# A delta-rule attention with two feed-forward nets on one core: stage 0 with six banks and an order of its own, part of the weight work on GpSimd, and group 1's columns in stage 1

## The reference

```python
k_n = k / (np.linalg.norm(k, axis=-1, keepdims=True) + 1e-06)
for t in range(S):                       # B, H, S, D = 4, 8, 768, 48
    kt, vt, bt = (k_n[:, :, t], v[:, :, t], beta[:, :, t, None])
    y[:, :, t] = np.einsum('bhd,bhde->bhe', q[:, :, t], state)
    v_old = np.einsum('bhde,bhd->bhe', state, kt)
    state = state + bt[:, :, :, None] * np.einsum('bhd,bhe->bhde', kt, vt - v_old)
...
h = np.maximum(x @ w_in, 0.0)            # x: 3072 tokens x 384, w_in: 384 x 2048
x = h * h @ w_out                        # w_out: 2048 x 384
...
gate = 1.0 / (1.0 + np.exp(-(x @ w_gate)))
val = x @ w_val                          # 384 x 1536 each
return gate * val @ w_out                # 1536 x 384
```

## Time and profile before

| | |
|---|---|
| device time, three runs | 1011.26 us median (1009.72 to 1011.65) |
| profiled execution | 1009.18 us |
| its span, from the first to the last instruction | 1007.4 us |
| PE busy | 959.8 us, 95% of the span |
| DVE, ACT, POOL busy | 543.9, 481.2, 13.3 us |
| mean granted TensorE clock, as a share of full speed | 0.974 |

### The profile page before, as it was taken

One profiled execution on the slowest core, in us unless ns is written; L12 is line 12 of the kernel. 1 busy time (PEld: TensorE's weight loads), 2 busy tenths in 40 slices (PEclk: granted clock), 3 DMA queues, 4 the chain that ended last, 5 costly groups with the idle time before them and its releaser, 6 DMA issues.

```text
span 1007.4 us, 23469 instructions
## 1 busy us (share of the span) xinstructions
PE 959.8 (95%) x10030; PEld 490.9 (49%) x10030; DVE 543.9 (54%) x1075; ACT 481.2 (48%) x865; POOL 13.3 (1%) x27
## 2 busy tenths in 40 slices
PE   2876999999999999999999999999999999999997
PEld 1463565565565456546544444444444444444443
DVE  7979957947857885793335532523423423424322
ACT  4875575756576477555669732232222222221321
POOL 0000000000000000000000000000000000000000
PEclk7868999999999999999999999999999999999999
DMA  9516016015005202202033010010100100100000
GB/s 312 120 35 127 2 34 128 33 49 113 33 4 109 50 34 65 64 33 77 21 126 126 1 63 1 0 62 0 62 0 0 62 0 0 62 0 0 31 0 31
DMA packets 20708, 52.16 MB, mean 52 GB/s; under 512 B 2640, under 2 KB 12880, under 8 KB 20240
## 3 DMA queue, kind: packets, MB, share of 16 engines
q1 hardware_dynamic: 20032, 50.60, 17.8%
q10 hardware_dynamic: 592, 0.33, 0.2%
HBM read 41.48 MB, written 9.44 MB: 51 GB/s over the span
## 4 chain that ended last, share of the span: by engine, by line
PE 87%; DVE 6%; ACT 2%; issue 2%; DMA 1%; SPq 0%; POOL 0%; DVEq 0%; POOLq 0%
PE psum L641 75%; PE psum L555 2%; PE psum L499 1%; PE psum L486 1%; DMA raw_a<-in_w_in 1%; PE psum L512 1%; PE psum L524 1%; DVE attn L1086 1%; PE psum L542 1%; ACT w L822 1%; PE psum L570 1%; PE psum L584 1%; DVE work L1127 1%; PE psum L451 1%; DVE attn L1066 1%
## 5 line engine op out<-in xcount | busy, mean ns | idle before, releaser
L641 PE MATMUL psum<-work,attn 128*128 128x512 f16 x1944 | 419.9, 379 | 0.1
L641 PE MATMUL psum<-work,w 128*128 128x512 f16 x1728 | 386.3, 380 | 9.7 <-issue 5.9
L641 PEld LDWEIGHTS psum<-work,attn 128*128 128x128 f16 x1944 | 190.1, 98 | 229.7 <-DVE work L1127 0.6
L641 PEld LDWEIGHTS psum<-work,w 128*128 128x128 f16 x1728 | 164.2, 98 | 204.5 <-issue 9.5
L728 ACT ACTIVATE work<-work 128x512 f16<-128x512 f32 (+1 forms) x264 | 155.7, 624 | 142.9 <-DVE work L1260 139.9
L1260 DVE SCALAR_TENSOR_TENSOR work<-psum,work 128x512 f32<-128x512 f32 x72 | 49.8, 692 | 271.4 <-PE psum L641 261.8
L728 ACT ACTIVATE work<-psum,scal 128x512 f32<-128x512 f32 x90 | 60.5, 686 | 169.9 <-PE psum L641 169.9
L1108 DVE SCALAR_TENSOR_TENSOR work<-work 128x512 f16<-128x512 f16 x96 | 66.1, 690 | 61.5 <-ACT work L728 59.8
L728 ACT ACTIVATE attn<-psum 64x384 f32<-64x384 f32 (+5 forms) x160 | 65.9, 441 | 65.8 <-PE psum L512 34.7
L728 ACT ACTIVATE work<-psum 128x512 f32<-128x512 f32 x96 | 57.2, 595 | 64.3 <-PE psum L641 63.0
L1066 DVE TENSOR_TENSOR attn<-attn 128x31 f32<-128x31 f32 (+15 forms) x186 | 63.8, 343 | 6.4
(11 more groups left out here) (97 smaller groups left out, 558.5 us busy)
## 6 DMA issues: line engine op xcount, KB each, us to landing
attn<-in_kt SPq DMA_DIRECT2D x24, 192.0 KB, 4.2
attn<-in_v SPq DMA_DIRECT2D x24, 192.0 KB, 4.6
attn<-in_kn SPq DMA_DIRECT2D x24, 192.0 KB, 3.8
x_spill<-work SPq DMA_DIRECT2D x6, 768.0 KB, 3.4
xt<-x_spill SPq DMA_DIRECT2D x6, 768.0 KB, 5.0
y_out<-work SPq DMA_DIRECT2D x6, 768.0 KB, 3.6
attn<-in_qt SPq DMA_DIRECT2D x20, 192.0 KB, 4.1
work<-in_w_out SPq DMA_DIRECT2D x1, 3072.0 KB, 23.7
```

Of the source, the lines that this page charges most:

```text
L641: m = mm(dst, x, z, start=first and i == 0, stop=last and i == len(a) - 1)
```

## The change

Stage 0 gets a table of its own. The pool has six banks there instead of three: the three further ones are PSUM banks 2, 3 and 4, which the pieces of `w_in` and later the outputs use too (`a_bank`, `PIECE_SHARED`). A bank goes to a fill by longest rest, and the read-out of three fills is put later than the fill (`READ_LATER`). The 12 pieces of `w_in` go four by four into the same four banks, with group 1's Grams of keys between them. `cut_out` and `cut_small`, eight instructions, go from ACT to GpSimd. `place_e` is done by halves. The maximum of x is taken chunk by chunk, and ACT makes the high part of group 0's x. `start` of stage 0 is 35, so that `coefficients`, `start_lanes` and all 31 columns of group 1 come behind `split_x`. `keep_clock` stands behind certain fills (`WARM_BEHIND`) instead of ahead of them.

```diff
+NB_FIRST = 6
...
-    0: dict(mid=(2, 2), off=(8, 15), qk=(7, 19), ks=(-7, 14), dr=(13, 20), grow=(14, 25), xt=(14, 28), xmax=28, xscale=31, xsplit=31, kk=(0, 0), lanes=5, norm=6, start=8, small=(3, 7, 17, 17), hi_out=(0, 4, 8, 9), first_out=(7, 8, 19, 21)),
+    0: dict(kk=(0, 1), qk=(2, 9), mid=(3, 5), off=(4, 7), dr=(6, 13), grow=(8, 14), ks=(-7, 10), xt=(11, 15), lanes=3,
+            norm=3, root=12, xmax=16, xscale=17, xsplit=18, start=35, place_e=(3, 8), first_out=(5, 7, 13, 13), first_max=13),
...
+READ_LATER = {("qk", 0, 1, 0): 12, ("qk", 0, 1, 1): 12, ("off", 0, 0, 1): 9}
...
+    _n = NB_FIRST if _s == 0 and (_kind, _g) != ("kk", 1) else NB
+    _b = min(range(_n), key=lambda b: _last[b])
...
-REST_BANK, REST_PIECES = (2, 3, 4, 1, 5, 6, 7, 2, 3, 4, 1, 2), 12
-REST_FIRST = 12
+REST_PIECES = 12
+REST_BANK = (1, 3, 4, 2) * 3
+REST_AT = {OPEN: (0, 1, 2, 3), 0: (4, 5, 6, 7), 1: (8, 9, 10, 11)}
...
+WARM_BEHIND = {("mid", 0, 0): 4, ("mid", 1, 1): 1, ("dr", 1, 1): 4, ("su", 1, 1): 2, ("xt", 1, 1): 14}
...
-        a_bank = [psum[:, b, :] for b in (5, 6, 7)]
+        a_bank = [psum[:, b, :] for b in (5, 6, 7, 2, 3, 4)]
...
             def open_fill(*f):
 
+                if f in PIECE_SHARED:
+                    pe.wait_ge(w_lo_done, REST_PIECES)
...
+            def first_high_parts():
+
+                act.wait_ge(x_scaled, 5)
+                act.wait_ge(w_small_done, W_PIECES)
+                act.wait_ge(w_out_done, W_PIECES)
+                for kc in range(KC):
+                    run(x_hi[:, kc], xt32[:, TOK * kc:TOK * (kc + 1)], scale=cell(X + 2)).then_inc(x_cut, 1)
...
+            def cut_out(n):
+
+                at = slice(part // W_PIECES * n, part // W_PIECES * (n + 1))
+                nc.gpsimd.tensor_scalar(w1h[:, 2 * part:3 * part][:, at], raw_o[:, at], cell(WO + 2), None, ALU.mult)\
+                    .then_inc(w_out_hi, 1)
...
             all_of(wsq_part, wsq_all, 2, WO, RADD)
+            pool.wait_ge(w_step, W_STEPS * 2)
+            for n in range(W_PIECES):
+                cut_out(n)
+            pool.wait_ge(small_scaled, 1)
+            for n in range(W_PIECES):
+                cut_small(n)
...
+            def max_of_chunk(c):
+
+                for x in range(2):
+                    wait_taken(dve, "xt", 0, c, x)
+                link(V.tensor_reduce(scal[:, 32 + KC * c:32 + KC * (c + 1)],
+                                     xt32[:].rearrange("p (k c f) -> p k c f", k=KC, c=NC)[:, :, c], AX.X, ALU.max,
+                                     apply_absolute_value=True), xmax_first, c + 1)
```

More of the change, by code:

```diff
@@ L116, in other_work @@
 def other_work(s, step):
-    us = sum(EVACUATION.get(kind, 0.0) for kind, *_ in FILL_AT.get((s, step), []))
+    us = sum(EVACUATION.get(kind, 0.0) for kind, *_ in READ_AT.get((s, step), []))
     for name, cost in (("rows", 4.3), ("scale_v", 3.2), ("xmax", 1.8), ("xscale", 1.0), ("xsplit", 4.0), ("lanes", 2.2),
@@ L622, in attention @@
                         turn(g, c, x)
+                    if s == 0:
+                        keep_clock(WARM_BEHIND.get((kind, c if kind not in ("mid", "off") else x, x), 0) if g == 0 else 0)
             def rest_of_first(n):
@@ L678, in stage @@
                     attention(s, step)
[L679 to L683, removed]
+                    if s == 0:
+                        for n in REST_AT.get(step, ()):
                             rest_of_first(n)
@@ L891, in stage @@
                     if 0 < s < GROUPS and step == place(s, "rows") + 1:
-                        place_e(s)
-                    for f in FILL_AT.get((s, step), []):
+                        place_e(s, slice(0, UN), NC)
+                    for f in READ_AT.get((s, step), []):
                         evacuate(*f)
+                    if s == 0 and step in place(0, "place_e"):
+                        c = place(0, "place_e").index(step)
+                        place_e(0, slice(PAIRS * c, PAIRS * (c + 1)), 1)
+                    if s == 0 and step == place(0, "xsplit"):
+                        first_high_parts()
                     if s == 0 and step == OPEN:
@@ L905, in stage @@
                         weight_root(1, WO)
-                        for n in range(REST_FIRST):
+                    if s == 0:
+                        for n in REST_AT.get(step, ()):
                             cut_rest_first(n)
-                    if s == 0 and step == 0:
-                        place_e(0)
-                    for n in range(REST_FIRST, REST_PIECES):
-                        if s == 0 and step == place(0, "rest")[n - REST_FIRST]:
-                            cut_rest_first(n)
-                    for n in range(W_PIECES):
-                        if s == 0 and step == place(0, "hi_out")[n]:
-                            cut_out(n)
-                        if s == 0 and step == place(0, "small")[n]:
-                            cut_small(n)
-                    if s < GROUPS - 1 and step == place(s, "norm"):
+                    if s < GROUPS - 1 and step == place(s, "norm" if s else "root"):
                         root_k(s + 1)
@@ L1203, in stage @@
                         scale_v(s)
-                    for f in FILL_AT.get((s, step), []):
+                    for f in READ_AT.get((s, step), []):
                         evacuate(*f)
+                    if s == 0 and step == place(0, "first_max"):
+                        max_of_chunk(0)
                     if chain and step == place(s, "xmax"):
```

68 lines of the change are left out of this document (39 added, 29 removed).

## The result

The changed kernel takes 1030.1 us (median of 4 runs, 1029.2 to 1031.2) where the kernel before took 1010.7 beside it: a ratio of 1.0183, 95% interval 1.0171 to 1.0195. It is slower, as I had said, but by 19.5 us and not by 4, and it lies outside my range. The profiled execution has a span of 1026.4 us and a time of 1030.21, so 3.8 us lie outside its span, where it was 1.8 before; the three other executions have spans of 1027.2 to 1029.1 us. Medians that are compared with this kernel's therefore differ by some 2 us more than the fixed points in the traces do.

The account below looks back on a forecast made before the run. PE (TensorE) was taken as the bound, busy nearly throughout, so only an earlier F pays: -4.5 + 8.25 = +3.8 us on the profiled 1009.2 gives 1013.0, with 2.1 to the median 1015; range 1008.5 to 1024.

Parts of the forecast that it names:

- F: Start of TensorE's first hidden block, 93.18 us in the kernel before; forecast at 88.7 us, a gain of 4.5.
- Term 2: Stage 1, behind F: 11.2 us of VectorE's coefficients and columns move there, making TensorE wait 8.25 us.
- The wait for the keys and its cold clock: Stage 0: TensorE idles 5.9 us from 32.3 for group 1's keys, then half clock costs 3.3 us, between 0 and 4.
- Rival A: At 38 us in stage 0 the clock costs nothing: F = 85.4, 1011.7 us, no change; chance 0.19.
- The parts that cost nothing: Stage 0: GpSimd's eight pieces at 1.6 us each, between 1.43 and 3.6, decide only above 5.6; ACT's relief and six banks add nothing.
- Rival B: Stage 0: GpSimd's reads each stop one VectorE column; F = 91.7, 1018 us, or 1024 at 2.2 us each; chance 0.28.
- term 1: Stage 0 walk along PE's and DVE's new order: F = 85.4, or 88.7 with 3.3 us for the clock.
- Rival C: Stage 0: PE not held at group 1's keys; F = 82.7, 1009.1 us; chance 0.16 with a too-long walk added.

Follow-up runs that it names:

- experiment 1: The changed kernel with the eight pieces of w_out back on ScalarE (ACT) instead of GpSimd; 1020.25 us, ratio 1.0092.
- experiment 3: experiment 1 with group 1's coefficients and first nine columns back in stage 0; 1012.32 us, ratio 1.0009.
- experiment 8: The changed kernel with each of GpSimd's eight pieces written as two instructions of 768 elements; 1029.08 us, ratio 1.0173.
- experiment 7: experiment 3 with the edits of experiment 5 and experiment 6 together; 1006.54 us, ratio 0.9948.
- experiment 6: experiment 3 with 19 more zero products ahead of chunk 1's first products, where TensorE stands still at 70 us; 1010.17 us, ratio 0.9989.
- experiment 5: experiment 3 with group 1's keys loaded ahead of values, queries and the k*s keys in SP's queue; 1008.76 us, ratio 0.9973.
- experiment 4: The kernel before with the eight pieces of w_out on GpSimd and the small scale made earlier; 1035.72 us, ratio 1.0242.
- experiment 10: experiment 7 with halved pieces on GpSimd, an idle all-reduce behind them, group 1's lanes cleared between the two sets; 1008.48 us, ratio 0.9979.

## Why the prediction was wrong, point by point

The sign was right and the size was not: 8.25 us of debt were there, and the gain of 4.5 ahead of F was a loss of 10.7.

- **Term 2, the debt of 8.25 us: right.** 8.3 in the changed kernel, 7.9 from experiment 1 to 3. The first `project` starts at F + 11.1, forecast as F + 11.2, and the block behind group 1's first `mid` at F + 39.4, forecast as about 40. How the time is spent differs: the wait ahead of that `project` is 3.4 us and not 5 to 6, because the three hidden blocks ahead of it ran cold and ended at F + 7.7 and not at F + 5.9. The added waits are 6.2 us (5.3 for the low parts, 0.9 for the attention), and the first five blocks take 1.9 us longer than before (13.07 us for 11.16).
- **The wait for the keys and its cold clock: right.** The keys' products began at 39.16 and not 38.2, and the first `qk` started at 55.72 where the walk, with the clock's 3.3 us, has 51.5 + 3.3 = 54.8: 0.9 late, all of it from the keys. Rival A (no cost of the clock) is out.
- **"The parts that cost nothing" is the step that failed.** It priced the pieces at 1.6 us within 1.43 to 3.6 and said that they decide only above 5.6. They took 4.3 to 4.5, outside both bounds and still under 5.6, and the price was not what mattered. What did was a cost that I had not on the list: changing GpSimd to another kind of instruction and back, 6.4 to 7 us each in this kernel, the second time between the maximum of x and the split. It put 6.65 us on F; the holds put 1.2 there. Without the pieces the change takes 1020.25 us (experiment 1), still 5 us over the forecast; that rest is the walk and the second cold stretch, below.
- **Rival B** had the mechanism right (VectorE held by GpSimd's reads) and the victims only in part. It had each piece stop one column; in fact one column, the scaling of v, one small instruction of one input, and the first two of the four low pieces of `w_out` were held, for longer each, and the path saw 1.2 us and not 6.3 to 12.5. The Trainium skill's page "SBUF — State Buffer", section "Who interferes with whom", says that the engine that comes second is blocked until the other's instruction is done, for VectorE instructions with two SBUF inputs and also for `tensor_scalar` in a two-port mode. The traces agree, with 3.26 us for 60 elements and 2.16 for a TENSOR_SCALAR of 32 that takes 0.19 alone (whether this one ran in such a mode no view shows); experiment 8 agrees on the length.
- **The walk itself, term 1, was too short by 4.2 us.** With no cold stretch on the way and no pieces on GpSimd (experiment 7) it is 90.91 - 52.84 = 38.1 us from the first `qk` to F, where my walk has 85.4 - 51.5 = 33.9. Of this, 2.0 are two `qk` fills, which I took at 1.1 us like the other kinds and which take 2.08 at full clock; the other 2.2 are spread over the steps behind. That every fill costs 1.1 was a choice, and no row of `qk` was read for it, though the trace of the kernel before has one at full clock:

```profile
75.36 2.08 PE L486 MATMUL psum<-attn 48*64 48x64 f32 x64
```

- **The second cold stretch was missing: 2.2 us** (experiment 6). My walk had a wait ahead of `qk` of chunk 1 and did not ask what it does to the clock, though it asked exactly that at the keys.
- **Rival C**, keys early, as a kernel of its own gave F 3.5 us earlier than experiment 3 (experiment 5), where my numbers have 6.0 (88.7 less 82.7): it had the eight pairs run at full clock without a break, and the first of them ran cold, behind TensorE's wait of 2.0 us for ScalarE.

Together: 0.9 for the keys, 4.2 for the walk, 2.2 for the clock, 6.65 for the code load and 1.2 for the holds make 15.15 of the 15.2 us between 88.7 and 103.87. That it closes is no proof of its own, since most terms are differences from one experiment to the next. The 1.2 and the 2.2 come from pairs of single profiled executions, whose first `qk` differ by up to 0.5 us, so each may be off by some tenths. Not tried: the order of before with six banks and nothing else, so what the banks alone bring stays open.

## What to carry to other kernels

Work moved to GpSimd has four prices, and only the first is in the instruction's own row: its duration, the hold of VectorE's instructions beside it (cut the pieces small), the change of its code before and behind (put an idle instruction of the next kind right behind the work, where there is time), and whatever stands behind it in its queue (the clearing of the lanes). What each costs depends on how near VectorE is to the path: the holds cost F 1.2 us in the changed kernel and most of 18 in experiment 4. When a wait is found on a walk, ask at each one, not only at the first, what the clock does behind it, and price each kind of fill by a row of its own kind. Columns that fill idle time before the bound engine starts should stay there: moved behind it they cost their full 8 us.

## What the runs showed of the hardware

- GpSimd's change from the all-reduce to a TENSOR_SCALAR took 6.7 to 7.6 us, and back 5.7 to 6.5 (six traces each). The timeline shows it only as idle time put down to "issue"; the view of a line's instructions has a pair of MODIFY_POOL_CONFIG at its start. The change to its MEMSET (78.49, right behind a piece) cost nothing and has no such pair.
- A TENSOR_SCALAR of GpSimd of 128x1536 elements, f32 to f16, takes 4.15 us at the shortest and 4.3 to 4.5 on the mean of four; ScalarE's takes 1.5. With VectorE busy with many short instructions it was longer: 19.2 and 19.6 us for four pieces in experiment 10, against 17.7 in experiment 8.
- The granted clock fell to 0.50 behind waits of TensorE of 5.1 and 2.5 us, and in experiment 5 behind one of 2.0; it stayed at 1.00 through one of 2.5 us in experiment 10 (76.6 to 79.1). Eleven zero products of 0.23 us each in the wait at 70 us kept it at 1.00 in experiment 6.
